# Two ScalarE jobs moved in time and one pair of tiles computed from sums and differences, in a three-stage kernel on one Trainium2 core

## The chip, the cores and the metric

The kernel runs on one core of one Trainium2 chip. Time is device time in microseconds (us) of one execution; lower is better. The engines are named as in the profile: PE is TensorE's matmuls and PEld its weight loads, DVE is VectorE, ACT is ScalarE, POOL is GpSimd, SP is SyncE, which issues most of the DMAs. L731 is line 731 of the kernel before.

## The reference, cut to what matters

Four batches, each of 768 tokens by 384 columns (8 heads of 48), go through three steps.

```python
state = alpha[:, :, t, :, None] * state + einsum('bhd,bhe->bhde', k[:, :, t], v[:, :, t])   # a recurrence over tokens
y[:, :, t] = einsum('bhd,bhde->bhe', q[:, :, t], state)

X = np.fft.fft(np.fft.fft(x, axis=1), axis=2)        # over tokens, then over columns
u = x + np.real(X)
un = (u - mean(u)) / sqrt(var(u) + 1e-6)
x2 = u + relu(un @ w_ch1) @ w_ch2                    # 384 -> 1536 -> 384

h = relu(x2.T @ w_tok1) @ w_tok2                     # token mixing, 768 -> 256 -> 768
u2 = x2 + h.T
out = u2 + relu(u2 @ w2_ch1) @ w2_ch2
```

## The kernel before

Every fp32 product is made of three matmuls of rounded parts (`three`: high by high, high by low, low by high), so each operand is split into a high part (ACT) and a low part (DVE or POOL).

**Stages.** A batch is processed in order: 24 visits of the attention (4 units of two heads each, 6 chunks of 128 tokens in a unit), a tail with the Fourier transform and the normalisation, and 48 slots of the first MLP. The visits and the tail of batch b + 1 are interleaved by hand, slot by slot, with the MLP of batch b: at slot h an engine first does its MLP work, then `visit(b + 1, VISITS[b][h])`, then `tail(b + 1, h)`. Only batch 0 has its visits and its tail alone. After batch 3 a second phase does the token mixing and the second MLP batch by batch. Every engine has its own program, written out in the order in which it executes; waits are on semaphores, and nothing overtakes on an engine.

**Attention and the range test.** A unit's queries, keys and decays arrive as one DMA of 1011.5 KB into `qkap` (`load_unit`, L445); for units 2 and 3 of a later batch SP issues it once visit 5 or visit 11 is done. In visit k ACT copies the queries of chunk k + 2 (`attn_qz`, L689), the turned keys (`attn_krt`, L682), the result of chunk k (`attn_x`, L695) and half of the decayed state (`decay`, L702). ACT also tests once for each unit whether any decay lies above or below two limits (`range_of`, L710; `out_of_range`, L731, for batch 0): two ACTIVATEs over 112 x 768 elements with a running sum. DVE needs both sums before it overwrites the decays of that unit's first chunk (`prep_prefix`, L942). For batches 1 to 3, unit n + 1 is tested in visit k = 6n + 2:

```python
if a and k > 0 and k % NC == 2 and k // NC + 1 < NU:
    for i in range(2):
        range_of(a, k // NC + 1, i)
```

**Tail.** DVE folds the batch's `x` into `xf`, ACT and DVE split that into `xh` and `xl` (`split_x`, L764 and L1142), and PE makes six Fourier tiles over the tokens (`f1`), which are split into `gh` and `gl` (`split_g`, L770 and L1146). PE also turns three tiles of `x` with a permutation (`flips`, L1514); ACT copies them into the odd tiles of `us` (`copy_flipped`, L751), and then two single rows (`first_edge_rows`, L756, batch 0 only). In batch 0 these copies stand in ACT's program behind the third `split_g`, at slot `FLIPS_AT = 35`.

The second Fourier step gives for each of three pairs of tiles two products of 194 columns, V (`f2_v`) and U (`f2_u`). PE's order is V0, U0, the middle row, V1, U1, V2, U2. ACT copies V to `vs` (`copy_v`, L778). The even tile of a pair is x - V + U and the odd one is flipped x + V + U in the first 193 columns; in the other 191, which read V and U backwards, the signs of V change. For the first pair DVE adds V to both tiles (`fourier_v`, four instructions of some 193 columns, L1155) and then U to both at once (`fourier_u`, two instructions of 2 x 193, L1170). For the other two pairs POOL adds V and DVE adds U. `fourier_middle` (L1177) writes one row of tile 1, `norm_stats` and what follows normalise the tiles into `un` (L1221, L792), PE turns them (`norm`, L1573), and the MLP starts. While batch 0's normalisation runs, PE executes a fixed number of dummy matmuls (`fill`, L1626; `FILL = {44: 10, 46: 4}`).

Of the kernel before, what the change touches and what calls it, by code (L numbers as in the profile page):

```python
# [7 lines left out]
ALU = mybir.AluOpType  # L8
ACT = mybir.ActivationFunctionType

P = 128
# [3 lines left out]
NC = S // P  # L15
# [35 lines left out]
RANGE_AT = {6: (2, 0), 7: (2, 1), 10: (3, 0), 12: (3, 1), 13: (0, 0), 14: (0, 1), 15: (1, 0), 17: (1, 1)}  # L51
RANGED = (6, 8, 2, 4)
TEST_AT = 20
FLIPS_AT = 35
FILL_TO, FILL_COL = 5, 384
VISITS = [dict(zip([h for h in range(31) if h not in pauses], range(-2, STEPS))) for pauses in PAUSES] + [{}]
SUMS_AT = 31
# [34 lines left out]
def program(nc, qka, v, v_sizes, w_ch1, w_ch2, w_tok1, w_tok2, w2_ch1, w2_ch2, dft, cs, mask_in, ident_in, flip_in, col_in, out):  # L92
    base = 16512

    def sb(name, shape, offset, dtype=F32):
        return nc.alloc_sbuf_tensor_at(name, shape, dtype, offset=base + offset)
# [72 lines left out]
    ext = sb("ext", [P, 4, NU], o); o += 64  # L169
    bad = sb("bad", [P, 2], o); o += 32  # L170
    spare = sb("spare", [P, 2], o); o += 32
    limits = sb("limits", [P, 2], o); o += 32
    flag = sb("flag", [1, 1], o, mybir.dt.int32); o += 32
    assert base + o <= 229344, base + o - 229344
# [34 lines left out]
    def sem(name):  # L209
        return nc.alloc_semaphore(name)  # L210
# [13 lines left out]
    s_suf, s_inv, s_pre, s_qk, s_qz, s_krt, s_sc, s_at, s_st, s_vis, s_x = map(  # L224
        sem, ["suffix_done", "inverse_ready", "prefix_done", "qk_ready", "qz_ready", "krt_ready", "scores_done",
              "at_ready", "state_ready", "visit_done", "x_ready"])
    s_dec = [sem(f"state_decayed{h}") for h in range(2)]

    s_ext, s_bad, s_badp, s_flag, s_rl, s_rc, s_rd, s_ry, s_rx = map(
        sem, ["ext_ready", "bad_ready", "bad_summed", "flag_ready", "rec_loaded", "rec_step", "rec_row_done",  # L230
              "rec_y_stored", "rec_x_loaded"])

    s_xs, s_fold, s_xhi, s_xlo, s_gp, s_ghi, s_glo, s_v, s_uv, s_vc, s_v0, s_pv, s_ua = map(
        sem, ["xsum_ready", "folded", "x_hi", "x_lo", "g_done", "g_hi", "g_lo", "v_done", "u_done", "v_copied",
              "v_added0", "v_added", "u_added"])

    s_bs, s_bn, s_ve, s_sd, s_unT, s_nhi, s_nlo = map(
        sem, ["bn_stats_done", "bn_aggr_done", "var_ready", "std_ready", "un_transposed", "n_hi", "n_lo"])
# [7 lines left out]
        sem, ["x2_hi", "x2_lo", "z_done", "z_hi", "z_lo", "mixed", "mixed_read", "u2_ready", "u2_transposed", "u2_hi",  # L246
              "u2_lo"])

    UA = 10
    DVE_TILES = (0, 2, 3)  # L250
    X2_PRIMED, MID_PRIMED, L2_PRIMED, OUT_PRIMED, FIN_PRIMED = NC, 32, 4, 32, NC
    MIX_BANKS = (5, 6, 7, 2, 3, 4)
# [150 lines left out]
    def v_bank(a, j):  # L403

        return bank[(5, 5, 7)[j] if a else (6, 2, 5)[j]]
# [15 lines left out]
    def v_terms(a, t):  # L421

        n, j = DM // 2 + 1, t // 2
        w, u = vs[:, j % 2, :], us[a % 2]
        src, ops = (u[:, t], (ALU.add, ALU.subtract)) if t % 2 else (x[:, j], (ALU.subtract, ALU.add))
        yield u[:, t, 0:n], src[:, 0:n], w[:, 0:n], ops[0]
        yield u[:, t, n:DM], src[:, n:DM], w[:, n - 2:0:-1], ops[1]

    with nc.Block() as block:
# [239 lines left out]
        def _(act):  # L669
# [65 lines left out]
            def visit(a, k):  # L735
                for h in range(2 if a else 0):
                    attn_qz(a, k + 2, h)
                attn_krt(a, k + 2)
                if k >= 0:
                    attn_x(a, k)  # L740
                decay(a, k + 2)
                if a and k > 0 and k % NC == 2 and k // NC + 1 < NU:
                    for i in range(2):
                        range_of(a, k // NC + 1, i)

            def copy_flipped(a):
                if a >= 2:
# [5 lines left out]
            def first_edge_rows():  # L753

                act.wait_ge(s_flipc, 3)
                act.activation(us[0][0:1, 3:6:2, :], x[0:1, 5:3:-1, :], ACT.Copy).then_inc(s_rows, 1)  # L756

            def split_x(a, step):
                for i in ((0, 1), (2,), (3, 4, 5))[step]:
                    t, part = f1_tile(i), i // KT  # L760
                    act.wait_ge(s_fold, a * 10 + (2, 4, 5, 8, 10, 10)[i])
                    m = slice(t * P, (t + 1) * P)
                    rows_ = slice(part * KT, (part + 1) * KT)
                    act.activation(xh[:, rows_, m], xf[:, rows_, m], ACT.Copy).then_inc(s_xhi, 1)  # L764

            def split_g(a, i):
                act.wait_ge(s_gp, a * (2 * KT) + i + 1)
# [4 lines left out]
            def copy_v(a, j):  # L772
                act.wait_ge(s_v, a * 3 + j + 1)
                if j == 2:
                    act.wait_ge(s_v0, a * 4 + 4)
                elif a:
                    act.wait_ge(s_pv, a * 8)
                act.activation(vs[:, j % 2, :], v_bank(a, j)[:, 0:FW], ACT.Copy,  # L778
                               scale=col[:, 0:1] if j == 0 else 1.0).then_inc(s_vc, 1)


# [19 lines left out]
            def tail(a, h):  # L801
                if h == SUMS_AT and a:
                    copy_flipped(a)
                if 0 <= h - SUMS_AT < 3:
                    split_x(a, h - SUMS_AT)
                if 0 <= h - F1_AT < 2 * KT:
                    split_g(a, h - F1_AT)
                if a == 0 and h == FLIPS_AT:
                    copy_flipped(0)
                    first_edge_rows()  # L810
                if h == STD_AT:
                    std(a, 0)
                if h == STD_AT + 1:
                    norm_rows(a, 1)
                if h in V_AT:
                    copy_v(a, V_AT[h])
                for t in NORM_AT.get(h, ()):
                    norm_split(a, t)
                if h == NEXT_AT + 1 and a + 1 < B:
                    first_range(a + 1)  # L820
# [85 lines left out]
        def _(dve):  # L906
# [241 lines left out]

            def fourier_v(a):

                dve.wait_ge(s_rows, a + 1)
                dve.wait_ge(s_vc, a * 3 + 1)
                for t in range(2):
                    for dst, src, w, op in v_terms(a, t):
                        dve.tensor_tensor(dst, src, w, op).then_inc(s_v0, 1)  # L1155

            def fourier_u(a, first, n, i):

                half, j = DM // 2 + 1, first // 2
                rows_ = us[a % 2][:, first:first + n, :]  # L1160
                uu = u_bank(a, j)[:, None, 0:FW].to_broadcast([P, n, FW])
                dst, src = ((rows_[:, :, 0:half], uu[:, :, 0:half]),
                            (rows_[:, :, half:DM], uu[:, :, half - 2:0:-1]))[i]
                if i == 0:
                    if j:
                        dve.wait_ge(s_pv, a * 8 + 2 * (first + n - 2))
                    else:
                        dve.wait_ge(s_v0, a * 4 + 4)
                    dve.wait_ge(s_uv, a * 4 + (1, 3, 4)[j])
                dve.tensor_tensor(dst, dst, src, ALU.add).then_inc(s_ua, 1)  # L1170

            def fourier_middle(a):

                n, u = DM // 2 + 1, us[a % 2]
                dve.wait_ge(s_uv, a * 4 + 2)
                dve.wait_ge(s_ua, a * UA + 2)
                dve.tensor_tensor(u[0:1, 1, 0:n], middle_bank(a)[0:1, 0:n], x[0:1, 3, 0:n], ALU.add).then_inc(s_ua, 1)  # L1177
                dve.tensor_tensor(u[0:1, 1, n:DM], middle_bank(a)[0:1, n - 2:0:-1], x[0:1, 3, n:DM], ALU.add
                                  ).then_inc(s_ua, 1)

            def norm_stats(b, t):

                dve.wait_ge(s_ua, b * UA + (2, 4, 6, 8, 10, 10)[t])
                dve.bn_stats(stats[:, t, :], us[b % 2][:, t, :]).then_inc(s_bs, 1)

            def norm_var(b, g):
# [43 lines left out]
            def tail(a, h):  # L1230
# [19 lines left out]
                    edge_rows(a)  # L1250
                if h == 40:
                    fourier_v(a)
                    for i in range(2):
                        fourier_u(a, 0, 2, i)
                if h == MIDDLE_AT:
                    fourier_middle(a)
                    norm_stats(a, 0)
# [166 lines left out]
        def _(pe):  # L1424
# [111 lines left out]
            def f2_v(a, j):  # L1536
                if j == 0:
                    pe.wait_ge(s_glo, a * (2 * KT) + 2 * KT - 1)
                elif a == 0:
                    pe.wait_ge(s_flipc, 3)  # L1540
                elif j == 1:
                    pe.wait_ge(s_vc, a * 3 + 1)
                else:
                    pe.wait_ge(s_ua, a * UA + 4)
                m = slice(j * P, (j + 1) * P)
                sums(v_bank(a, j)[:, 0:FW], ((2, m, 2), (3, m, 3))).then_inc(s_v, 1)

            def f2_u(a, j):
                if j == 0:
                    pe.wait_ge(s_glo, (a + 1) * (2 * KT))  # L1550
                elif j == 1 and a:
                    pe.wait_ge(s_ua, a * UA + 2)
                elif j == 2 and a:
                    pe.wait_ge(s_vc, a * 3 + 2)
                m = slice(j * P, (j + 1) * P)
                sums(u_bank(a, j)[:, 0:FW], ((0, m, 0), (1, m, 1))).then_inc(s_uv, 1)
# [4 lines left out]
            def norm(b, t):  # L1561

                if t == 0:
                    pe.wait_ge(s_ua, b * UA + (8 if b else 4))
                elif t == 1:
                    pe.wait_ge(s_vc, b * 3 + 3 if b else 1)
                elif t == 2:
                    pe.wait_ge(*((s_nlo, b * NC + 1) if b else (s_vc, 2)))
                elif t > 2:
                    pe.wait_ge(s_nlo, b * NC + t)  # L1570
                pe.wait_ge(*un_ready(b, t))
                for k in range(KT):
                    mm = pe.transpose(norm_bank(b, t)[:, k * P:(k + 1) * P], un[:, t % 3, k * P:(k + 1) * P],  # L1573
                                      ident[:, :])
                mm.then_inc(s_unT, 1)
# [228 lines left out]
```

## Time and profile before

| | us |
|---|---|
| median of 3 runs | 893.28 |
| the three runs | 890.87, 893.28, 893.49 |
| the profiled execution | 890.61 |
| its span (first to last instruction) | 888.8 |
| PE busy in the span | 875.4 |
| PEld / DVE / ACT / POOL busy | 846.9 / 437.6 / 326.6 / 189.8 |

Busy times are sums over the whole span, whose stages have different limits; the granted TensorE clock is 1.00 of full speed (2.4 GHz) throughout. A time of the rows below is a start from the beginning of the span.

### The profile page before, as it was taken

How to read it: one execution, taken by the hardware profiler on the slowest of the kernel's cores; microseconds unless marked ns; L12 is line 12 of the kernel's file. 1: busy time of each engine (PE TensorE's matmuls, PEld its weight loads, DVE VectorE, ACT ScalarE, POOL GpSimd, SP SyncE). 2: the span in 40 equal slices, each digit the busy share in tenths (PEclk: the TensorE clock that was granted, in tenths of full speed). 3: DMA queues.
4: the chain of work that ended last, by engine and by line, in shares of the span. 5: the costliest groups of instructions: out<-in, count | busy, mean ns of one | idle time of the engine just before them, and what ended most of it. 6: DMA issues, size and time to landing. Idle time of an engine off the chain costs nothing.

```text
span 888.8 us, 14640 instructions
## 1 busy us (share of the span) xinstructions
PE 875.4 (98%) x5386; PEld 846.9 (95%) x5386; DVE 437.6 (49%) x1078; ACT 326.6 (37%) x843; POOL 189.8 (21%) x321
## 2 busy tenths in 40 slices
PE   8999999999999999999999999999999999999998
PEld 6789889999999999999999999999999999999998
DVE  6778867567766577675542253222432142214121
ACT  2865674335654246653224332211221122112111
POOL 4733444023332024330113402000200020002000
PEclk9999999999999999999999999999999999999999
DMA  9961220040220412200072011000100010000000
GB/s 213 327 185 33 61 61 28 1 121 28 68 55 28 106 41 62 61 22 7 1 251 88 27 54 55 1 28 27 53 0 27 27 53 0 27 27 0 0 27 27
DMA packets 15002, 51.23 MB, mean 58 GB/s; under 512 B 1489, under 2 KB 6385, under 8 KB 13009
## 3 DMA queue, kind: packets, MB, share of 16 engines
q1 hardware_dynamic: 14368, 47.35, 17.9%
q0 software_dynamic: 576, 3.15, 0.9%
q8 instruction: 31, 0.51, 0.2%
q14 instruction: 27, 0.21, 0.1%
HBM read 41.07 MB, written 9.44 MB: 57 GB/s over the span
## 4 chain that ended last, share of the span: by engine, by line
PE 87%; DVE 4%; ACT 3%; DMA 2%; issue 2%; SPq 1%; DVEq 0%; POOL 0%; ACTq 0%
PE bank L1427 13%; PE bank L1429 13%; PE bank L1428 13%; PE pair L1427 12%; PE pair L1428 12%; PE pair L1429 12%; PE pair L1445 3%; PE bank L1464 3%; DMA qkap<-qka 2%; PE bank L1473 2%; PE pair L1454 1%; PE bank L1573 1%; ACT tested L731 1%; PE bank L1626 1%; PE bank L1434 1%
## 5 line engine op out<-in xcount | busy, mean ns | idle before, releaser
L1289 DVE SCALAR_TENSOR_TENSOR hl<-bank,hh 128x384 fp32r<-128x384 f32 x192 | 106.8, 556 | 332.7 <-ACT hh L825 332.5
L825 ACT ACTIVATE hh<-bank 128x384 fp32r<-128x384 f32 x192 | 94.3, 491 | 337.2 <-PE bank L1429 336.8
L1427 PE MATMUL bank<-nh,w1h 128*128 128x384 f32 x288 | 101.8, 353 | 0.2
L1427 PE MATMUL pair<-w2h,hh 128*128 128x384 f32 x288 | 101.2, 351 | 0.2 <-DVE u L1170 0.2
L1427 PE MATMUL bank<-u2h,w3h 128*128 128x384 f32 x288 | 97.0, 337 | 0.9 <-DVE u2l L1383 0.9
L1427 PE MATMUL pair<-w4h,hh 128*128 128x384 f32 x288 | 97.2, 338 | 0.0
L1428 PE MATMUL pair<-w4l,hh 128*128 128x384 f32 x288 | 97.0, 337 | 0.0
L1428 PE MATMUL pair<-w2l,hh 128*128 128x384 f32 x288 | 96.8, 336 | 0.0
L1429 PE MATMUL pair<-w2h,hl 128*128 128x384 f32 x288 | 96.8, 336 | 0.0
L1429 PE MATMUL bank<-nh,w1l 128*128 128x384 f32 x288 | 96.8, 336 | 0.0
L1428 PE MATMUL bank<-nl,w1h 128*128 128x384 f32 x288 | 96.8, 336 | 0.0
L1428 PE MATMUL bank<-u2l,w3h 128*128 128x384 f32 x288 | 96.6, 335 | 0.0
L1429 PE MATMUL bank<-u2h,w3l 128*128 128x384 f32 x288 | 96.6, 335 | 0.0
L1429 PE MATMUL pair<-w4h,hl 128*128 128x384 f32 x288 | 96.2, 334 | 0.0
L665 POOL TENSOR_TENSOR u<-u,x2l 128x384 f32<-128x384 f32 x24 | 23.6, 1014 | 275.0 <-DVE u L1404 275.0
L577 POOL TENSOR_TENSOR qkap<-qkap,suf 112x128 f32<-112x128 f32 (+1 forms) x81 | 39.8, 492 | 119.8 <-DVE suf L930 109.3
L689 ACT ACTIVATE qz<-qkap 48x128 f32<-48x128 f32 x144 | 44.2, 307 | 40.2 <-POOL qkap L587 37.8
L1427 PEld LDWEIGHTS bank<-u2h,w3h 128*128 128x128 f32 x288 | 54.1, 188 | 2.1 <-issue 2.1
L1427 PEld LDWEIGHTS bank<-nh,w1h 128*128 128x128 f32 x288 | 54.3, 189 | 1.4 <-DVE hl L1289 0.4
L1427 PEld LDWEIGHTS pair<-w2h,hh 128*128 128x128 f32 x288 | 54.3, 189 | 0.7 <-DVE u L1170 0.5
L1428 PEld LDWEIGHTS bank<-nl,w1h 128*128 128x128 f32 x288 | 54.2, 188 | 0.4
L1428 PEld LDWEIGHTS pair<-w2l,hh 128*128 128x128 f32 x288 | 54.3, 188 | 0.0
(201 smaller groups left out, 1838.0 us busy)
## 6 DMA issues: line engine op xcount, KB each, us to landing
qkap<-qka SPq DMA_DIRECT2D x15, 1011.5 KB, 7.6
vt<-v SPq DMA_DIRECT2D x16, 288.0 KB, 7.9
raw_a<-w_ch SPq DMA_DIRECT2D x6, 768.0 KB, 10.7
mid<-u SPq DMA_DIRECT2D x8, 576.0 KB, 2.8
raw_b<-w_ch SPq DMA_DIRECT2D x6, 768.0 KB, 6.3
out<-u SPq DMA_DIRECT2D x8, 576.0 KB, 2.8
xr<-mid SPq DMA_DIRECT2D x7, 576.0 KB, 3.8
raw_t<-w_tok SPq DMA_DIRECT2D x2, 768.0 KB, 6.0
```

The lines of the kernel that those rows point to most:

```text
L577: pool.tensor_tensor(keys.rearrange("p (c n) -> p c n", n=P), keys.rearrange("p (c n) -> p c n", n=P), after.rearrange("p (c n) -> p c n", ...
L665: pool.tensor_tensor(u2[:, t, :], u2[:, t, :], x2l[:, t, :].bitcast(F32), ALU.add).then_inc(s_u2, 1)
L689: act.activation(qz[head_rows(h), k % 2, h, :], q_of(a, k, head_rows(h)), ACT.Copy).then_inc(s_qz, 1)
L731: act.activation(tested[0:PR, :].rearrange("p (c n) -> p c n", n=P), decays(src), ACT.Relu, scale=(1.0, -1.0)[i], bias=limits[0:PR, i:i + ...
L825: act.activation(hh[:, s % 4, :], bank[s % 2][:, 0:HALF], ACT.Relu).then_inc(s_hhi, 1)
L1289: dve.scalar_tensor_tensor(out=hl[:, s % 4, :], in0=bank[s % 2][:, 0:HALF], scalar=0.0, in1=hh[:, s % 4, :].bitcast(F32), op0=ALU.max, op1 ...
L1427: pe.matmul(out_ap, wh, rh, start=first, stop=False)
L1428: pe.matmul(out_ap, wh, rl, start=False, stop=False)
L1429: return pe.matmul(out_ap, wl, rh, start=False, stop=last)
L1445: return pe.matmul(score_bank(a, k)[:, 0:2 * P], k_of(a, k), qz[0:PR, k % 2, :, :].rearrange("p h t -> p (h t)"), start=True, stop=True)
L1464: mm = pe.matmul(y[:, h * D:(h + 1) * D], at[:, k % 2, h, :], vb[:, c, h * D:(h + 1) * D], start=h == 0, stop=c == 0 and h == 1)
L1473: mm = pe.matmul(y, q_of(a, k), dec[0:PR, k % 3, :], start=False, stop=True)
```

## The change

Three edits:

1. **Range tests.** The two tests of unit n + 1 are made in two visits, the first in visit k = 6n + 1 and the second in visit 6n + 2 (batches 1 to 3).
2. **Flipped copies of batch 0.** `copy_flipped(0)` moves to between the third and the fourth `split_x` on ACT, and `first_edge_rows` to between the fourth and the fifth.
3. **First pair of tiles, all batches.** DVE waits for U0 and for the copy of V0, writes the difference U - V to `vs[:, 1]` and the sum U + V to a new buffer `both`, waits for both, and adds each half tile once: four instructions. `fourier_u(a, 0, 2, i)` goes. V1 is now copied to `vs[:, 0]` after the difference and the sum are made; PE waits for these two (`s_diff`) before V1 and U1 in batches 1 to 3 and before the first `norm` in batch 0. The count of `s_ua` for a batch grows from 10 to 12, and the waits on it change accordingly.

```diff
-FLIPS_AT = 35
...
-    UA = 10
+    UA = 12
...
-        w, u = vs[:, j % 2, :], us[a % 2]
+        w, u = vs[:, j // 2, :], us[a % 2]
...
-                if a and k > 0 and k % NC == 2 and k // NC + 1 < NU:
-                    for i in range(2):
-                        range_of(a, k // NC + 1, i)
+                if a and k > 0 and k % NC in (1, 2) and k // NC + 1 < NU:
+                    range_of(a, k // NC + 1, k % NC - 1)
...
                     act.activation(xh[:, rows_, m], xf[:, rows_, m], ACT.Copy).then_inc(s_xhi, 1)
+                    if a == 0 and i == 2:
+                        copy_flipped(0)
+                    if a == 0 and i == 3:
+                        first_edge_rows()
...
                 if j == 2:
-                    act.wait_ge(s_v0, a * 4 + 4)
+                    act.wait_ge(s_ua, a * UA + 4)
+                elif j == 1:
+                    act.wait_ge(s_diff, a * 2 + 2)
                 elif a:
                     act.wait_ge(s_pv, a * 8)
-                act.activation(vs[:, j % 2, :], v_bank(a, j)[:, 0:FW], ACT.Copy,
+                act.activation(vs[:, j // 2, :], v_bank(a, j)[:, 0:FW], ACT.Copy,
...
-                if a == 0 and h == FLIPS_AT:
-                    copy_flipped(0)
-                    first_edge_rows()
...
             def fourier_v(a):
+                n, u, u0 = DM // 2 + 1, us[a % 2], u_bank(a, 0)[:, 0:FW]
+                diff, total = vs[:, 1, :], both[:, :]
+                dve.wait_ge(s_vc, a * 3 + 1)
+                if a:
+                    dve.wait_ge(s_pv, a * 8)
+                dve.wait_ge(s_uv, a * 4 + 1)
+                for dst, op in ((diff, ALU.subtract), (total, ALU.add)):
+                    dve.tensor_tensor(dst, u0, vs[:, 0, :], op).then_inc(s_diff, 1)
+                dve.wait_ge(s_diff, 2 * a + 2)
                 dve.wait_ge(s_rows, a + 1)
-                dve.wait_ge(s_vc, a * 3 + 1)
-                for t in range(2):
-                    for dst, src, w, op in v_terms(a, t):
-                        dve.tensor_tensor(dst, src, w, op).then_inc(s_v0, 1)
+                for t, src, left, right in ((0, x[:, 0], diff, total), (1, u[:, 1], total, diff)):
+                    dve.tensor_tensor(u[:, t, 0:n], src[:, 0:n], left[:, 0:n], ALU.add).then_inc(s_ua, 1)
+                    dve.tensor_tensor(u[:, t, n:DM], src[:, n:DM], right[:, n - 2:0:-1], ALU.add).then_inc(s_ua, 1)
...
                     fourier_v(a)
-                    for i in range(2):
-                        fourier_u(a, 0, 2, i)
...
                 elif j == 1:
-                    pe.wait_ge(s_vc, a * 3 + 1)
+                    pe.wait_ge(s_diff, a * 2 + 2)
...
                 elif j == 1 and a:
-                    pe.wait_ge(s_ua, a * UA + 2)
+                    pe.wait_ge(s_diff, a * 2 + 2)
...
                 if t == 0:
-                    pe.wait_ge(s_ua, b * UA + (8 if b else 4))
+                    pe.wait_ge(*((s_ua, b * UA + 10) if b else (s_diff, 2)))
                 elif t == 1:
-                    pe.wait_ge(s_vc, b * 3 + 3 if b else 1)
+                    pe.wait_ge(*((s_vc, b * 3 + 3) if b else (s_diff, 2)))
```

## Rows read from the trace of the kernel before

**Rows 1.** Windows: stretch, its length, then each engine's busy us (instructions), clock.

```profile
core 0 of [0], span 888.8 us
78.00:160.00 82.00, 79.48 (x511) 75.07 (x510) 60.51 (x166) 49.38 (x151) 33.71 (x66) 1.00 0.14 41
203.00:285.00 82.00, 81.96 (x532) 78.86 (x531) 57.32 (x163) 48.29 (x148) 29.24 (x66) 1.00 0.17 48
```

**Rows 2.** Waits of PE: who waited for whom, us in total, times, longest.

```profile
PE pair L1445 <- DVE st L917: 2.3, 2, 1.5
PE bank L1427 <- DVE gl L1146: 1.5, 1, 1.5
```

**Rows 3.** Timeline of ACT, batch 0's tail: start, us, instruction [idle before, releaser].

```profile
53.47 0.53 ACT L764 ACTIVATE xh<-xf 128x384 fp32r<-128x384 f32 x1 [1.51 <-DVE xf L1122]
55.09 0.94 ACT L764 ACTIVATE xh<-xf 128x384 fp32r<-128x384 f32 x2 [1.09 <-DVE xf L1112]
...
56.75 1.26 ACT L751 ACTIVATE u<-pair 128x384 f32<-128x384 f32 x3
58.05 0.84 ACT L756 ACTIVATE u<-x 1x768 f32<-1x768 f32 x1
58.80 0.70 ACT L770 ACTIVATE gh<-bank 128x384 fp32r<-128x384 f32 x2
```

**Rows 4.** Timeline of DVE and PE between the two Fourier steps of batch 0.

```profile
59.32 0.82 DVE L1146 TENSOR_TENSOR gl<-bank,gh 128x384 fp32r<-128x384 f32 x2 [1.64 <-ACT gh L770]
60.19 0.36 PE L1427 MATMUL bank<-csh,gh 128*128 128x194 f32 x1 [1.54 <-DVE gl L1146]
60.95 0.28 PE L1427 MATMUL bank<-csh,gh 128*128 128x194 f32 x1
```

**Rows 5.** Timeline of DVE and PE from the second Fourier step to the normalisation.

```profile
61.68 0.63 DVE L1155 TENSOR_TENSOR u<-x,vs 128x193 f32<-128x193 f32 x2 [1.27 <-ACT vs L778]
62.88 1.02 DVE L1170 TENSOR_TENSOR u<-u,bank 128x386 f32<-128x386 f32 x2
64.83 4.50 PE L1626 MATMUL bank<-mask,ident 128*128 128x256 f32 x20
65.46 0.59 DVE L1170 TENSOR_TENSOR u<-u,pair 128x193 f32<-128x193 f32 x2
68.56 0.86 DVE L1221 TENSOR_SCALAR un<-u,mv,nrm 128x384 f32<-128x384 f32 x2
```

**Rows 6.** Timeline of ACT and PE around batch 1's test of unit 1 (visit 2).

```profile
88.86 0.84 ACT L675 ACTIVATE w2h<-raw_a 128x768 fp32r<-128x768 f32 x1
90.39 0.64 ACT L689 ACTIVATE qz<-qkap 48x128 f32<-48x128 f32 x2 [0.69 <-POOL qkap L587]
91.85 0.94 ACT L710 ACTIVATE tested<-qkap,limits 112x768 f32<-112x768 f32 x1
92.97 0.94 ACT L710 ACTIVATE tested<-qkap,limits 112x768 f32<-112x768 f32 x1
93.90 0.47 ACT L825 ACTIVATE hh<-bank 128x384 fp32r<-128x384 f32 x1
...
95.61 0.67 PE L1445 MATMUL pair<-qz,qkap 112*128 112x256 f32 x2 [0.81 <-DVE st L917]
```

**Rows 7.** Timeline of ACT and PE around batch 1's test of unit 2 (visit 8).

```profile
108.92 0.64 ACT L689 ACTIVATE qz<-qkap 48x128 f32<-48x128 f32 x2 [1.32 <-POOL qkap L587]
111.12 0.94 ACT L710 ACTIVATE tested<-qkap,limits 112x768 f32<-112x768 f32 x1
115.49 0.67 PE L1445 MATMUL pair<-qz,qkap 112*128 112x256 f32 x2 [1.47 <-DVE st L917]
```

**Rows 8.** DMA: issue of unit 2 in batch 1, its us to landing; all unit loads.

```profile
100.22 0.33 SPq L445 DMA_DIRECT2D qkap<-qka  x1
...
qkap<-qka SPq DMA_DIRECT2D x1, 1011.5 KB, 6.9
DMA to landing us min/median/max: 6.2/7.6/21.7
```

## Prediction before the run

> **What bounds the kernel now.** I read the windows by stage first. In a batch whose visits run under another batch's MLP, PE is busy 81.96 of 82 us, and DVE, ACT and POOL are far from full [rows 1]: there the end moves only if PE gets less work or if something makes it wait. The change gives PE the same matmuls, so it can win only where PE idles today. Batch 1's visits, under batch 0's MLP, show 79.48 busy of 82 us [rows 1], some 2.5 us idle.
>
> The waits of PE come next, because they say who ends that idle time. Two of them matter here: PE's scores waiting twice for the attention state of DVE (2.3 us, the longer 1.5), and the second Fourier step of batch 0 waiting 1.5 us for the low parts of DVE [rows 2]. These are the only places that the three edits can reach, 3.8 us in all.
>
> The timelines say what lies behind each wait. In the tail of batch 0, ACT copies the flipped tiles and the two rows from 56.75 to 58.89, and only then starts the fourth split of the Fourier tiles, at 58.80 [rows 3]; DVE's low parts follow at 59.32, and PE, idle 1.54 us, starts V0 at 60.19 [rows 4]. So the releaser named by the wait, DVE, is late because ACT was busy with copies that nobody needed yet. In batch 1's visit 2, ACT runs two tests from 91.85 and reaches the MLP's `hh` only at 93.90 [rows 6]. DVE's program has the low part of `hh` ahead of the next visit's state, so DVE idles with it and PE starts its scores at 95.61 after 0.81 us of idling. Visit 8 repeats this: the tests start at 111.12 and PE idles 1.47 us before 115.49 [rows 7].
>
> **The flipped copies.** Three copies cost 1.26 us and the two rows 0.84 [rows 3]; nothing is added or removed, they move. Their new places are the gaps in which ACT waits for DVE's folds: 1.51 us idle before the fourth `xh` at 53.47, and 1.09 us idle before the last two, of which the first starts at 55.09 [rows 3]. The copies leave 0.25 us of the one and the rows 0.25 us of the other, so I cost the new places at nothing. If that cover went, the overrun would fall on the splits and then on the first Fourier step; some 0.3 us at each place is my bound.
>
> What it gives: with ACT free at 56.75, the fourth and fifth splits follow the third at once (0.70 us for two, then 0.82 us on DVE [rows 3, 4]), which would put their low parts near 58.3. PE leaves the first Fourier step at 60.19 - 1.54 = 58.65 [rows 4], so V0 no longer waits for them. What is late next is U0, which needs the sixth split: ACT 0.70 / 2 = 0.35 behind 58.65, DVE 0.82 / 2 = 0.41, some 0.05 between them, so 59.45. Before, U0 started at 60.95 [rows 4]. The gain is 60.95 - 59.45 = 1.50 us. Its bounds are 0.9 (both overruns) and 1.64 (the whole wait, and what pipelining adds).
>
> Does the gain reach the MLP? The next fixed thing on PE is the dummy matmuls, 4.50 us from 64.83 [rows 5], which move with PE and end at 67.8. The normalised tile must be there by then. Today it is written from 68.56, two tiles in 0.86 us [rows 5], so the first at 68.99. DVE's chain has to move by at least some 1.2 us.
>
> **Sums and differences.** Before, DVE did two pairs of additions of V from 61.68 to about 62.85, and then U for both tiles in 1.02 us from 62.88 to 63.90 [rows 5]. After, two instructions that read U0 from PSUM and four in SBUF. The nearest rows are 0.59 us for a pair of 193 columns with PSUM, and 0.63 for a pair without [rows 5]. U0's last matmul starts at 59.45 + 0.63 (five steps of 0.76 / 6 = 0.127 us, the spacing of V0's six [rows 4]) and ends 0.28 later, 60.36. Then 0.59, a wait on itself of about 0.05, and 1.20 for two pairs as they stand today (61.68 to 62.88 [rows 5]): 62.2, which is 1.7 us earlier than 63.90. Left as it was, with V0 copied 1.6 us earlier, the old order would end at about 62.85 - 1.6 + 1.02 = 62.3. So this edit is worth about nothing in the head: it trades one wide pair for a narrow one and loses the overlap with U0. The normalised tile comes at 68.99 - 1.7 = 67.3, half a microsecond ahead of the dummy matmuls. The 1.5 us hold.
>
> A rule speaks against six short instructions: the Trainium skill, "VectorE: DVE Perf Modes", section "The TRN2 errata", gives (N + 151) / 0.96 ns for an fp32 add and says that many small tiles pay the fixed part each. By that estimate six of 193 columns take 2.15 us instead of my 1.84, the tiles are done at 62.5, and the sum stays the same, since the dummy matmuls still end later. The row of 0.59 us for two shows them overlapping, so I take the row.
>
> In batches 1 to 3 the new waits sit on PE ahead of V1 and U1, and behind them the MLP's matmuls are queued. PE does a whole MLP slot between U0 and V1, and the six DVE instructions replace six; I take nothing (0 to 0.3 us for a batch).
>
> **The range tests.** Each test costs 1.12 us ahead of another test (91.85 to 92.97) and 0.93 ahead of something else (92.97 to 93.90) [rows 6]. Six tests of a batch remain six; one of each pair moves a visit ahead.
>
> Visit 1 of batch 1: ACT is free at 88.86. The test ends at 89.79, the weight split (0.84) at 90.63, and the queries' copy, which started at 90.39 after 0.69 us of idling, is 0.24 late [rows 6]. The second test starts at 92.09 and `hh` at 93.02 instead of 93.90, 0.88 earlier. PE's idling of 0.81 us goes entirely.
>
> Visit 7: ACT idles 1.32 us ahead of 108.92, so from 107.60 [rows 7]; the test fits in 0.93 us and delays nothing. What follows visit 8's test comes 1.12 us earlier, and of 1.47 us, 0.35 stay. The wait for the state comes twice in the whole run [rows 2], so visits 13 and 14 have nothing to give back, nor have batches 2 and 3 [rows 1]. Gain 0.81 + 1.12 = 1.93 us; bounds 1.1 (the later one alone) and 2.28 (both).
>
> The test of unit 2 now needs its load earlier. It was issued at 100.22 and landed 6.9 us later, at 107.12 [rows 8], 0.48 before 107.60. The Trainium skill, "DMA: Bandwidth & Descriptors", sections "Measured" and "Latency and other measured facts", gives 6.15 us for 1 MB and about 2 us of fixed cost. By this estimate it lands at 108.4, the test would be 0.8 us late and the queries' copy 0.4, and the sum would lose up to 0.4 us; the row of 6.9 us is nearer to this kernel.
>
> **The sum.** 1.50 + 1.93 + 0 = 3.4 us; by the bounds 2.0 to 3.9. Against its own time the profiled execution would take 890.61 - 3.4 = 887.2. The three runs shown have 890.87, 893.28 and 893.49, so an execution may lie at either of two levels 2.7 us apart. The forecast is the median's: 893.28 - 3.4 = 889.9.
>
> **Rivals.**
> - *One of the two gains fails.* Either the start of batch 0's MLP is held by something that doesn't move (a weight's low part, the dummy matmuls), or PE, without its pauses, meets DVE at the next busy stretch: DVE is idle just when PE is, and has 60.51 us of work in these 82 [rows 1]. That leaves 1.5 to 1.9 us: 891.6. For it speaks that DVE's normalisation and weight splits are bunched; against it, that in each pause PE and DVE stop and resume together.
> - *Late loads, slower.* ACT's queue is in order, and a test that waits for its DMA holds the queries' copy, `hh` and the next state behind it. From 7.8 us to landing on (108.92 - 0.93 - 100.22) it delays, and from about 8.9 it costs more than the 1.12 us gained. The median of all unit loads is 7.6 [rows 8]. At 10 us each of six loads would cost PE some 1.1 us more than today: -1.5 - 0.8 + 6.6 = +4.3, 897.6.
> - *The change doesn't do what it says:* the moved copies overrun into the splits and the head gains nothing, while the second visit's wait only moves to the first. 893.
>
> **Chances.** Forecast 0.58, one gain only 0.31, late loads 0.05, nothing 0.06. Range: from the lower level with the upper bound, 890.61 - 3.9 = 886.7, to the upper level with 0.9, 892.4. A measurement can tell about 0.3%, 2.7 us, from no change; 3.4 lies a little beyond it. Faster by more than that 0.60 (the forecast, and a little of the next), within 0.35, slower 0.05.
>
> **What the profile after would show.** The wait of L1427 for L1146 falls from 1.5 us to some 0.2, and U0 starts near 59.5. The three `u` copies stand at 52.0, the two rows at 54.0. The first MLP matmul comes 1.5 us earlier. PE's wait for the state falls from 2.3 to about 0.35 us, and the two tests of a unit stand in neighbouring visits. I am wrong if an ACT test has a DMA as its releaser, if the fourth `xh` starts later than 53.5, or if these waits go and the span doesn't follow.

## The result, and the profile after

| | before | after |
|---|---|---|
| median, us | 893.06 (4 runs) | 886.99 (4 runs) |
| lowest to highest | 890.87 to 893.49 | 886.67 to 887.29 |
| profiled execution: time, span | 890.61, 888.8 | 887.18, 885.4 |
| granted clock of the profiled execution | 1.000 | 0.999 |

The ratio after to before is 0.9937, with a 95% interval of 0.992 to 0.9954: faster by 0.63%. (Executions of over 905 us, all at a mean granted clock of 0.974 or less, are left out here and below.) The two profiled spans differ by 3.4 us, the forecast to the tenth; the medians differ by 6.1. So two things are to be explained: whether the 3.4 us came from where the prediction said, and where the other 2.7 came from.

First the waits of PE in the kernel after (who waited for whom, us in total, times, longest), beside [rows 2]:

```profile
PE bank L1433 <- DVE u2l L1389: 0.9, 4, 0.2
...
PE pair L1433 <- DVE u L1178: 0.5, 1, 0.5
...
PE pair L1451 <- DVE st L920: 0.4, 1, 0.4
```

The wait for the state fell from 2.3 us in two places to 0.4 in one. The wait of 1.5 us for the low parts, L1433 for L1149 in the new numbering, is no longer in the list. The windows of the same stages, beside [rows 1]:

```profile
78.00:160.00 82.00, 81.47 (x526) 77.25 (x525) 61.78 (x169) 49.54 (x150) 33.21 (x65) 1.00 0.14 41
203.00:285.00 82.00, 81.91 (x530) 78.64 (x530) 57.52 (x163) 46.59 (x144) 27.29 (x62) 1.00 0.16 48
```

Batch 1's visits now have PE busy 81.47 of 82 us instead of 79.48, like those of the later batches, where nothing changed.

The timeline of the tail of batch 0, ACT first, beside [rows 3]:

```profile
52.14 1.23 ACT L751 ACTIVATE u<-pair 128x384 f32<-128x384 f32 x3
53.75 0.53 ACT L764 ACTIVATE xh<-xf 128x384 fp32r<-128x384 f32 x1 [0.38 <-DVE xf L1125]
54.18 0.83 ACT L756 ACTIVATE u<-x 1x768 f32<-1x768 f32 x1
55.37 0.94 ACT L764 ACTIVATE xh<-xf 128x384 fp32r<-128x384 f32 x2 [0.36 <-DVE xf L1115]
...
57.95 0.35 ACT L774 ACTIVATE gh<-bank 128x192 fp32r<-128x192 f32 x1 [0.39 <-PE bank L1435]
```

The copies and the two rows stand in the gaps, and 0.38 and 0.36 us of each gap are left. The splits of the Fourier tiles now wait for PE, not for ACT's copies. Then PE and DVE in the same stretch, beside [rows 4, 5]:

```profile
58.65 0.27 PE L1435 MATMUL pair<-dfth,xl 128*128 128x192 f32 x1
58.76 0.36 PE L1433 MATMUL bank<-csh,gh 128*128 128x194 f32 x1
59.75 0.36 PE L1433 MATMUL bank<-csh,gh 128*128 128x194 f32 x1
60.77 0.36 DVE L1161 TENSOR_TENSOR vs<-bank,vs 128x194 f32<-128x194 f32 x1 [1.08 <-PE bank L1435]
...
62.24 0.35 DVE L1166 TENSOR_TENSOR u<-u,vs 128x191 f32<-128x191 f32 x1
63.72 4.50 PE L1632 MATMUL bank<-mask,ident 128*128 128x256 f32 x20
67.26 0.86 DVE L1229 TENSOR_SCALAR un<-u,mv,nrm 128x384 f32<-128x384 f32 x2
```

PE leaves the first Fourier step at 58.65 + 0.27 = 58.92, 0.27 us later than in the profile before, since this execution reached the tail later: ACT's first split of `xf` starts at 50.09 instead of 49.82. V0 follows without a wait at 58.76 (pipelined), U0 at 59.75, and the dummy products start at 63.72 instead of 64.83. With the 0.27 us set apart, they are 1.38 us earlier. The first `hh` of the MLP, in the kernel before and in the kernel after:

```profile
49.82 0.99 ACT L764 ACTIVATE xh<-xf 128x384 fp32r<-128x384 f32 x2 [0.58 <-DVE xf L1122]
73.75 0.49 ACT L825 ACTIVATE hh<-bank 128x384 fp32r<-128x384 f32 x1 [0.73 <-PE bank L1429]
...
50.09 0.99 ACT L764 ACTIVATE xh<-xf 128x384 fp32r<-128x384 f32 x2 [0.58 <-DVE xf L1125]
72.60 0.49 ACT L828 ACTIVATE hh<-bank 128x384 fp32r<-128x384 f32 x1 [0.73 <-PE bank L1435]
```

From the first split to the first `hh` it takes 23.93 us before and 22.51 after: 1.42 us less.

Last, batch 1's visits, ACT and PE, beside [rows 6, 7]; the tests of visits 7 and 8 are the two shown:

```profile
93.52 0.64 PE L1451 MATMUL pair<-qz,qkap 112*128 112x256 f32 x2
...
105.51 0.94 ACT L711 ACTIVATE tested<-qkap,limits 112x768 f32<-112x768 f32 x1
106.80 0.64 ACT L690 ACTIVATE qz<-qkap 48x128 f32<-48x128 f32 x2 [0.26 <-POOL qkap L588]
109.00 0.94 ACT L711 ACTIVATE tested<-qkap,limits 112x768 f32<-112x768 f32 x1
...
112.25 0.67 PE L1451 MATMUL pair<-qz,qkap 112*128 112x256 f32 x2 [0.37 <-DVE st L920]
```

The scores that wait for what visits 2 and 8 hold up are those that PE makes in visits 4 and 10. In visit 4 they start at 93.52 without a wait. The test of visit 7 ends before POOL releases the queries' copy, and of 1.47 us of idling ahead of the scores of visit 10, 0.37 are left.

A third place, which the prediction doesn't have, gains too. The tests of visit 14 held up a split of the normalised tiles in the same way, and the weight load of an MLP product waited for its low part, `nl`. This wait stands in the list of PEld, not in PE's. First that line and the product in the kernel before, then the product after:

```profile
PEld bank L1427 <- DVE nl L1227: 0.3, 1, 0.3
135.02 0.45 PE L1427 MATMUL bank<-nh,w1h 128*128 128x384 f32 x1
...
131.42 0.42 PE L1433 MATMUL bank<-nh,w1h 128*128 128x384 f32 x1
```

After, the line is no longer in PEld's list. From before to after, PE's work stands 1.14 us earlier ahead of visit 4's scores, 2.09 earlier with them (95.61 to 93.52), 3.24 with those of visit 10 (115.49 to 112.25), and 3.60 with this product: gains of 0.95, 1.15 and 0.36 us.

One test of the kernel after waits for its load, unit 3's of batch 3:

```profile
369.67 0.94 ACT L711 ACTIVATE tested<-qkap,limits 112x768 f32<-112x768 f32 x1 [0.34 <-DMA qkap<-qka]
```

PE's list has no wait from 340 to 410 us, so this one costs nothing.

### The profile page after: what moved, and what is told of

Read it like the earlier page. It is cut to its first block, busy times and chain, and to the rows that moved or that the text cites. A ratio compares the mean times of both kernels' runs of the same rounds, so it can differ in the third digit from the quotient of the medians.

```text
span 885.4 us, 14641 instructions
## 1 busy us (share of the span) xinstructions
PE 875.8 (99%) x5386; PEld 847.9 (96%) x5386; DVE 435.3 (49%) x1078; ACT 325.2 (37%) x843; POOL 189.6 (21%) x321
## 4 chain that ended last, share of the span: by engine, by line
PE 95%; ACT 2%; DVE 2%; issue 1%; DVEq 0%; POOL 0%
PE bank L1433 14%; PE bank L1435 14%; PE bank L1434 14%; PE pair L1433 13%; PE pair L1434 12%; PE pair L1435 12%; PE pair L1451 4%; PE bank L1470 3%; PE bank L1479 2%; PE pair L1460 2%; PE bank L1626 1%; PE bank L1579 1%; PE bank L1440 1%; ACT tested L732 1%; PE bank L1475 1%; PE bank L1632 1%
## 5 line engine op out<-in xcount | busy, mean ns | idle before, releaser
L1433 PE MATMUL bank<-nh,w1h 128*128 128x384 f32 x288 | 101.8, 353 | 0.0
L1433 PE MATMUL pair<-w2h,hh 128*128 128x384 f32 x288 | 101.2, 351 | 0.5 <-DVE u L1178 0.5
L1433 PE MATMUL bank<-u2h,w3h 128*128 128x384 f32 x288 | 97.0, 337 | 0.9 <-DVE u2l L1389 0.9
L1433 PE MATMUL pair<-w4h,hh 128*128 128x384 f32 x288 | 97.3, 338 | 0.0
L1433 PEld LDWEIGHTS bank<-u2h,w3h 128*128 128x128 f32 x288 | 54.1, 188 | 2.2 <-issue 2.2
L1433 PEld LDWEIGHTS pair<-w2h,hh 128*128 128x128 f32 x288 | 54.4, 189 | 1.0 <-DVE u L1178 0.8
L1433 PEld LDWEIGHTS bank<-nh,w1h 128*128 128x128 f32 x288 | 54.4, 189 | 0.7 <-issue 0.2
```

What stands on the lines that cost most here:

```text
L1433: pe.matmul(out_ap, wh, rh, start=first, stop=False)
```

## Experiments

**Each edit alone, and the first two together.** All against 28 runs of the kernel before (median 892.61).

The first edit:

```diff
-                if a and k > 0 and k % NC == 2 and k // NC + 1 < NU:
-                    for i in range(2):
-                        range_of(a, k // NC + 1, i)
+                if a and k > 0 and k % NC in (1, 2) and k // NC + 1 < NU:
+                    range_of(a, k // NC + 1, k % NC - 1)
```

> The kernel before with the first edit alone (the two tests of a unit in two visits). Theory (two waits of PE go, 1.5 us in batch 0's tail by the second edit and 1.9 us in batch 1's visits by the first): span 886.9, PE's wait for the state falls from 2.3 to about 0.4 us, the wait of 1.5 us for DVE's low parts stays. Rival A (the first edit only moves the wait to the neighbouring visit): span within 0.5 us of 888.8. Rival B (the 2.6 us by which the medians moved more than the spans come from this edit: the kernel before runs now at 890.7 and now at 893.3, and the later load or the double test makes the upper level): all runs lie in one level near 888.8 us, none near 891.4.

The second edit:

```diff
+                    if a == 0 and i == 2:
+                        copy_flipped(0)
+                    if a == 0 and i == 3:
+                        first_edge_rows()
...
-                if a == 0 and h == FLIPS_AT:
-                    copy_flipped(0)
-                    first_edge_rows()
```

> The kernel before with the second edit alone (the flipped copies and the two rows between the splits of x). Theory: span 887.3, PE's wait for DVE's low parts falls from 1.5 to 0.3 us, the wait for the state stays at 2.3. Rival A (without the third edit DVE's additions are late and the dummy matmuls no longer cover them): less than 1 us of gain. Rival B (this edit removes the upper level): all runs near 889.2, none near 891.8.

The third edit is the kernel after with these two undone.

```diff
-                if a and k > 0 and k % NC in (1, 2) and k // NC + 1 < NU:
-                    range_of(a, k // NC + 1, k % NC - 1)
+                if a and k > 0 and k % NC == 2 and k // NC + 1 < NU:
+                    for i in range(2):
+                        range_of(a, k // NC + 1, i)
...
-                    if a == 0 and i == 2:
-                        copy_flipped(0)
-                    if a == 0 and i == 3:
-                        first_edge_rows()
...
+                if a == 0 and h == FLIPS_AT:
+                    copy_flipped(0)
+                    first_edge_rows()
```

> The kernel before with the third edit alone (first pair of tiles from difference and sum). Theory: span within 0.3 us of 888.8, since the dummy matmuls end after the normalised tile either way. Rival A (the new waits hold V1 and U1 in batches 1 to 3): 0.5 to 2 us longer. Rival B (this edit removes the upper level): all runs near 890.7, none near 893.3.

Both of the first two, in the kernel before:

```diff
+                    range_of(a, k // NC + 1, k % NC - 1)
...
+                        copy_flipped(0)
...
+                        first_edge_rows()
```

> The first and the second edit together, without the third. Theory: span 885.4 within 0.3 us, as with all three. Rival A (the third edit carries a part of the head's gain): span 0.4 to 1.5 us longer than with all three. Rival B (the third edit removes the upper level): runs at two levels, 887 and 889.7.

| edits | median, us | ratio to before | 95% interval | spans of single runs (granted clock) |
|---|---|---|---|---|
| first | 890.07 | 0.9976 | 0.9966 to 0.9987 | one 886.1 (1.000); eleven 887.7 to 888.7 (0.997 to 0.998) |
| second | 890.50 | 0.9975 | 0.9964 to 0.9985 | five 887.3 to 888.0 (0.999 to 1.000); six 888.7 to 889.3 (0.997 to 0.998) |
| third | 892.87 | 1.0005 | 0.9997 to 1.0014 | twelve 890.7 to 892.0 (0.995 to 0.998) |
| first and second | 886.92 | 0.9939 | 0.9923 to 0.9956 | five 884.3 to 885.4 (0.999 to 1.000) |

Each of the first two edits removes the wait it should and leaves the other. PE's lists, two lines of the first edit and one of the second:

```profile
PE bank L1426 <- DVE gl L1145: 1.5, 1, 1.5
PE pair L1444 <- DVE st L916: 0.4, 1, 0.4
...
PE pair L1446 <- DVE st L918: 2.3, 2, 1.5
```

The first leaves 0.4 us of 2.3, the second leaves none of the 1.5. The third does nothing that these runs can tell from zero (none of its 12 runs is at full clock, which may be chance), and the first two do without it what all three do. The spans expected were 886.9, 887.3 and 888.8; at full clock the first two came out at 886.1 and at 887.3 to 888.0, but most runs lie above, and all of the third's. And 2.5 and 2.1 us make 4.6, but together they save 5.7. The last column has a pattern that no wait explains: a kernel with one of the two waits left runs at more than one level, and the higher level has the lower granted clock.

The profile of the third edit alone happened to be of such an execution (892.0, clock 0.995). Its windows around the two waits (stretch, length, busy us of PE, PEld, DVE, ACT, POOL, then the granted clock):

```profile
58.00:60.00 2.00, 0.61 (x6) 0.44 (x4) 0.73 (x2) 1.66 (x4) 2.00 (x2) 1.00 0.31 46
60.00:62.00 2.00, 1.85 (x12) 1.85 (x12) 0.36 (x2) 0.42 (x1) 0.34 (x1) 0.72 0.87 291
62.00:64.00 2.00, 2.00 (x12) 1.78 (x12) 1.47 (x6) 0.00 (x0) 0.00 (x0) 0.50 0.95 277
64.00:66.00 2.00, 2.00 (x18) 2.00 (x18) 1.86 (x6) 1.42 (x3) 0.94 (x2) 0.93 1.12 310
...
116.00:118.00 2.00, 0.97 (x7) 0.95 (x8) 1.86 (x7) 1.38 (x4) 0.41 (x1) 1.00 0.00 0
118.00:120.00 2.00, 2.00 (x11) 2.00 (x11) 1.93 (x7) 1.35 (x5) 1.24 (x3) 0.73 0.00 0
120.00:122.00 2.00, 2.00 (x9) 1.79 (x8) 1.39 (x2) 1.38 (x4) 1.04 (x1) 0.50 0.00 0
122.00:124.00 2.00, 2.00 (x15) 2.00 (x15) 1.68 (x5) 0.74 (x3) 0.55 (x2) 0.92 0.04 9
```

PE idles ahead of V0 in 58 to 60 at full clock, and right behind that pause the clock stands at 0.50, the 1.2 GHz level: PE is busy for 2.00 us in 62 to 64 and gets through 12 matmuls, against 18 in the next window. The same follows visit 8's pause, in 118 to 122. The pause is paid twice, once as idle time and once as slow matmuls behind it. The Trainium skill, "TensorE: Matmul & The Clock Gate", section "What's actually happening", has the throttled clock as the default that activity releases; these windows agree.

The 70 runs of the kernel before that were made beside those of this part fall into three groups:

| granted clock | runs | spans | median span |
|---|---|---|---|
| 0.999 to 1.000 | 17 | 888.0 to 889.7 | 888.6 |
| 0.997 to 0.998 | 34 | 890.1 to 892.5 | 890.8 |
| up to 0.996 | 19 | 891.3 to 892.7 | 891.7 |

The profiled execution of the kernel before belongs to the first group, which a quarter of its runs reach; the trace with two falls, 892.0 us long, has the clock of the third.

**Is it the clock?** A theory that rests on the pause can be tested without shortening it: keep the order of all work and fill PE's idle time with products that nobody reads. They go to a PSUM bank whose contents have been taken and which the next real product overwrites.

```diff
                 if j == 0:
+                    if a == 0:
+                        pe.wait_ge(s_glo, 2)
+                        for _ in range(3):
+                            pe.matmul(bank[6][:, 0:2 * P], ident[:, :], mask[:, None, :].to_broadcast([P, 2, P]), start=True, stop=True)
                     pe.wait_ge(s_glo, a * (2 * KT) + 2 * KT - 1)
```

> The kernel before, with three dummy products (six matmul records, about 1.3 us) on PE ahead of V0 of batch 0, where PE idles 1.5 us; nothing else is changed. Clock theory (behind a pause of PE the granted clock falls to half for some 3 us in most executions, and the change removed that too): the fall behind the tail no longer occurs, the fall behind visit 8 stays, so runs at about 890 and 891.5, median 891.2 against 892.6. Rival (the extra 2 us of the medians are shorter waits alone): same time as the kernel before, within 0.3 us, since the waits end where they ended.

```diff
                 if 0 <= k + 1 < STEPS:
+                    if a == 1 and k in (4, 10):
+                        s, n = {4: (5, 3), 10: (8, 6)}[k]
+                        pe.wait_ge(s_hlo, s)
+                        for _ in range(n):
+                            pe.matmul(bank[(s - 1) % 2][:, 0:P], ident[:, :], mask[:, :], start=True, stop=True)
```

> The kernel before, with the dummy products ahead of V0 and further ones (three and six products of 128 columns, 0.7 and 1.3 us) ahead of PE's scores in visits 4 and 10 of batch 1, where PE idles 0.8 and 1.5 us. Clock theory: no run falls, all near 890.3 (the kernel before's lowest level), 2.3 us under its median, with every wait of the change still there in length. Rival (waits alone): same as the kernel before, 892.6.

The first of these additions on top of the first edit, and the second on top of the second edit:

> The first edit (tests in two visits) and the dummy products ahead of V0. Clock theory: all runs at the level of the one undisturbed run of the first edit alone, 888.0, against its median of 890.1. Rival (the upper level of the first edit alone is another cause than the clock): 890.1.

> The second edit (flipped copies between the splits) and dummy products ahead of PE's scores in visits 4 and 10 of batch 1, where PE idles 0.8 and 1.5 us with the tests still in one visit. Clock theory: the second edit alone ran in two groups, spans of 887.3 to 888.0 at full clock and 888.7 to 889.3 with 0.997 to 0.998; with the dummies only the first group is left, median 889.5. Rival (the second group is another cause): two groups as before, median 890.5.

| kernel | median, us | ratio to before | 95% interval | spans (granted clock) |
|---|---|---|---|---|
| before + dummies ahead of V0 | 890.70 | 0.9979 | 0.997 to 0.9987 | twelve 888.0 to 889.5 (0.999 to 1.000) |
| before + dummies at both places | 890.79 | 0.9983 | 0.9974 to 0.9992 | twelve 888.4 to 889.5 (0.999 to 1.000) |
| first edit + dummies ahead of V0 | 887.98 | 0.9952 | 0.9937 to 0.9966 | six 885.9 to 887.7 (0.999 to 1.000) |
| second edit + dummies in visits 4, 10 | 889.45 | 0.9964 | 0.9948 to 0.998 | six 887.0 to 887.9 (0.999 to 1.000) |

(The kernel before has a median of 892.71 beside the first three and of 892.77 beside the fourth.) Of each kernel only executions at full clock are left. Filling the pause ahead of V0, with no other change, saves 2 us, which is the kernel before without its falls. On top of the first edit it saves another 2.1, on top of the second the visits' dummies save 1.0. So the extra time is the clock's.

The traces show the two prices side by side. The tail is taken from the first split of `xf` to the first `hh` of the MLP, batch 1's visits from there to the fifteenth `hh` (us):

| kernel | tail | batch 1's visits |
|---|---|---|
| before | 23.93 | 75.13 |
| third edit (two falls) | 25.51 | 76.73 |
| before + dummies ahead of V0 | 23.93 | 75.10 |
| before + dummies at both places | 23.93 | 75.11 |
| first edit | 23.92 | 72.63 |
| second edit (fall behind visit 8) | 22.50 | 76.72 |
| second edit + dummies in visits 4, 10 | 22.51 | 75.13 |
| first and second | 22.53 | 72.67 |
| after | 22.51 | 72.67 |

The dummies leave the length of both stages as it is, so the waits are not shortened. The second edit takes 1.4 us out of the tail, the first edit 2.5 out of the visits, and a fall adds 1.6 us to its stage.

One expectation failed: the dummies ahead of V0 should have left the fall behind visit 8, and none of 12 runs showed it; so the dummies in visits 4 and 10 had nothing left to gain there. The trace of that kernel, windows around visit 8's pause:

```profile
112.00:116.00 4.00, 2.63 (x18) 2.29 (x16) 1.61 (x5) 3.54 (x9) 1.02 (x3) 1.00 0.00 0
116.00:120.00 4.00, 3.88 (x26) 3.79 (x27) 3.79 (x11) 2.93 (x8) 2.50 (x5) 1.00 0.00 0
```

and the same windows of the second edit alone:

```profile
112.00:116.00 4.00, 2.51 (x17) 2.17 (x16) 2.77 (x8) 2.78 (x9) 1.01 (x3) 1.00 0.00 0
116.00:120.00 4.00, 4.00 (x18) 3.80 (x17) 3.07 (x8) 2.57 (x8) 1.69 (x3) 0.57 0.00 0
```

PE idles 1.49 us ahead of visit 10's scores in both, and only the second falls. The pause alone doesn't decide it, then; what does is left open.

**What does a late load cost?** The rival of late loads is tried by moving both tests one visit further ahead.

```diff
-                if a and k > 0 and k % NC in (1, 2) and k // NC + 1 < NU:
-                    range_of(a, k // NC + 1, k % NC - 1)
+                if a and k >= 0 and k % NC in (0, 1) and k // NC + 1 < NU:
+                    range_of(a, k // NC + 1, k % NC)
```

> The kernel after, with both tests a visit earlier still (visits 6n and 6n + 1), so that for units 2 and 3 the first one stands some 2 us before its load lands. Prices the rival of late loads. If a late load holds ACT as that rival says (each of six loads costs PE 1.1 us): 892 to 894. If the slack behind ACT takes it up: 887 to 888, with a DMA as releaser of the tests.

902.27 us, ratio 1.0109 (1.0091 to 1.0127), slower than both kernels; 892 to 894 were expected. Some waits of this kernel, PE's, and the DMA's part in those of ACT's tests:

```profile
PE pair L1451 <- DVE st L920: 3.9, 2, 2.4
PE bank L1579 <- DVE un L1229: 2.8, 2, 1.4
PE pair L1451 <- ACT qz L690: 1.8, 2, 1.0
...
PE pair L1451 <- DVE at L1061: 0.9, 2, 0.5
...
  DMA qkap<-qka: 16.7, 6
```

Six tests wait 16.7 us for their loads, 2.8 each, and the span is 898.5 instead of 885.4: 13.1 us, 2.2 for each load. PE waits in all three batches, behind the state, the normalised tiles and the queries: 3.9 + 2.8 + 1.8 + 0.9 = 9.4 us in these lines, 9.0 more than in the kernel after, 1.5 for each load. The clock falls with it (0.995), and the other 4 us are put down to that, though no run separates the clock from the tests' new places. In the kernel after, unit 2's load of batch 1 landed at 98.10 + 6.7 = 104.8, and the test started at 105.51, 0.7 us later. Unit 3's of batch 3 had no such room: issued at 362.85, landed 6.8 later at 369.65, and its test waited 0.34 us.

**Repeats, and a version meant to be better.** The kernel after, the first two edits, and the kernel after with nine dummy products, beside runs of the kernel before with a median of 892.50:

```diff
-FILL = {44: 10, 46: 4}
+FILL = {44: 9, 46: 4}
```

> The kernel after as it is, side by side with the two below. Theory: 887.0 us, every run at the full clock, 6 us under the median of the kernel before, of which 3.4 are the waits and the rest the clock.

> The first and the second edit without the third, beside the kernel after. Theory (the third edit does nothing for the time): within 0.3 us of the kernel after. Rival (its new chain is later, as the wait of 0.5 instead of 0.2 us for the last pair's additions suggests): 0.3 to 0.6 us faster than the kernel after.

> The kernel after with nine instead of ten dummy products while batch 0 is normalised. Theory (the dummy products end after the normalised tile and set the start of the turns, so they hold the MLP): 0.3 us faster, 886.7. Rival (the tile sets it): no change. Clock: a gap of 0.1 us is no reason to fall, so full clock in all runs.

The kernel after 886.77 us (0.9941, 0.9925 to 0.9957), the first two edits 886.72 (0.9943, 0.9927 to 0.9958), nine dummies 886.92 (0.9944, 0.9928 to 0.996). The three can't be told apart. The third edit adds nothing and costs nothing, though its wait for the last pair's additions is 0.5 us, against 0.2 without it. One dummy fewer gives nothing that the medians show; the 0.3 us expected didn't come. In its trace the tail takes 22.35 us, against 22.48 in the repeat of the kernel after, and 0.13 us is too little for six runs whose spans differ by 0.8 to tell.

## Why the prediction was right, and which term it lacked

*The flipped copies, 1.50 us.* Right in mechanism and nearly in size: the tail is 1.40 to 1.43 us shorter in the four traces of the table that have the edit. The gaps of ACT took the copies, with more room than the 0.25 us forecast. U0 starts at 59.75 - 0.27 = 59.48, forecast 59.45. The fourth `xh` starts at 53.75, later than the 53.5 that the prediction named as a sign of being wrong; with the 0.27 us by which this execution reached the tail later it is 53.48, so the copies didn't push it. Spans weigh this edit less well: the five runs of it alone at full clock have a median of 887.7, only 0.9 under the first group's 888.6. Where the tail begins, up to which these kernels don't differ, lies anywhere from 49.10 to 50.49 us in the traces, enough to hide half a microsecond.

*Sums and differences, nothing.* Right: 1.0005 alone, and no difference with and without it next to the other two. The tiles are done at 62.24 + 0.35 - 0.27 = 62.3, forecast 62.2, and the normalised tile comes before the dummy products end, as forecast.

*The range tests, 1.93 us.* Right in mechanism, too small: the visits are 2.46 us shorter (75.13 to 72.67). Visit 4 gave 0.95 instead of 0.81 and visit 10 gave 1.15 instead of 1.12. The other 0.36 us came from behind visit 14, which the prediction put at nothing ("visits 13 and 14 have nothing to give back") because it looked for the wait for the state alone, in the list of PE; the wait there was for `nl`, in the list of PEld.

*The sum, 3.4 us.* The terms make 1.42 + 2.46 = 3.9, the upper bound of the prediction. That the two profiled spans differ by 3.4 is luck: the execution after reached the tail 0.27 us later, and its stages behind the visits took 0.2 us longer in all.

*The median, 889.9.* Here a step failed. The prediction saw that an execution may lie "at either of two levels 2.7 us apart", took the levels for something that the change leaves alone, and carried the sum over to the median. The levels were the second price of the very pauses that the change removes. Of the 6.1 us, some 3.9 are the waits and 2.2 the clock. That fits the step from the first group to the second (888.6 to 890.8), in which the median run lies; a fall costs 1.6 us in the trace, and what makes up the rest of that step is open. From the second group to the third it is 0.9, so that two falls come to 3.1 by the groups and 3.2 by the trace. The profile could not show it, since the profiled execution was one of the quarter without a fall; the spread of 890.61 to 893.49 over runs of one kernel was the only hint. So the measured time lies in the range, but near its lower end, which was drawn from the lower level for another reason.

*Rivals.* Neither gain failed. One load was late, by 0.34 us and without a cost to PE, so the sign of being wrong that the prediction named, a test with a DMA as its releaser, is there once and harmless. The rival of late loads had the price of the waits about right: by its rule, the delay less 1.12, a delay of 2.8 us costs PE 1.7, and PE's waits grew by 1.5 for each load. What it lacked is most likely the clock again: the whole span grew by 2.2 for each. The first rival's fear, that PE and DVE would meet at the next busy stretch, is not seen: PE is busy 81.47 of 82 us with DVE at 61.78.

## What to carry to other kernels

A pause of PE of about 1.5 us can cost its length twice: look at the granted clock of single runs, not only of the profiled one, and read a spread in levels as a cost that hangs on something in the program. Where a pause can't be removed, filling it with products that nobody reads gave back 2 us here without touching any order. A long job on an in-order engine is best put into a gap in which that engine waits for something else anyway, and split where its two halves find two such gaps, as long as its data are there.

## What the runs showed of the hardware that was not expected

53 of 70 runs of the kernel before have a mean clock under 0.999, though PE's longest pauses in its trace are only 1.5 us long. Behind such a pause, with PE busy again, the clock was at 1.2 GHz for a stretch that cost 1.6 us, as long as the pause itself. The traces that show a fall have the clock at 0.50 in windows behind the pauses, not in them; of runs without a trace only the mean clock and the span tell of it. The fall behind visit 8 came, by these, in 6 of 11 runs of the second edit alone and in none of 12 with the pause ahead of V0 filled, although PE idles there as long. Which property of the earlier stretch decides that was not settled.
